# Local attention of a fused attention and feed-forward kernel, cut into blocks of 26 queries and 32 keys in place of 58 and 64

## The reference

```python
B, H, S, D = 4, 8, 576, 64; factor = 4
out_d = sm_attn(q_d, k_d, v_d)           # q, k, v averaged over groups of 4 rows: 144 positions
out_up = np.repeat(out_d, factor, axis=2)
mask = np.abs(pos[:, None] - pos[None, :]) < factor
scores = scale * np.matmul(q, k.transpose(0, 1, 3, 2))
scores = np.where(mask, scores, -1000000000.0)
attn = softmax(scores)                    # max taken off, exp, divided by the row's sum
out_local = np.matmul(attn, v)
return out_up + out_local
# then x (2304 tokens, 512 wide): h = x @ w_in (1024), h * softmax(h), layer norm * g_ln, @ w_out
# then h = x @ w_in2 (2048), h * cos(h), @ w_out2
```

## Time and profile before

| | us |
|---|---|
| median of three runs | 696.54 (693.97 to 698.17) |
| profiled execution, its own time | 697.5 |
| span of the profiled execution, first to last instruction | 695.7 |
| TensorE matmuls busy | 680.9 (98%) |
| VectorE, ScalarE, GpSimd busy | 440.8, 407.6, 233.3 |

### The profile page before, as it was taken

How to read it: one execution, slowest core, us unless ns; L and a number is a source line. 1 busy time by engine, 2 the same in 40 slices (tenths; PEclk the granted TensorE clock), 3 DMA queues, 4 the chain that set the end, 5 groups by cost and what they waited for, 6 DMA issues and landing times.

```text
span 695.7 us, 12769 instructions
## 1 busy us (share of the span) xinstructions
PE 680.9 (98%) x4783; PEld 601.3 (86%) x4783; DVE 440.8 (63%) x806; ACT 407.6 (59%) x849; POOL 233.3 (34%) x315
## 2 busy tenths in 40 slices
PE   7889999999999999999999999999999999999998
PEld 4567889889889999999898988888989898899986
DVE  7688964664662424266888888975555676655553
ACT  4558874664654665565666657564444676444444
POOL 6697864454542455411222255700000430000000
PEclk9999999999999999999999999999999999999999
DMA  8944222231300000537544343342222336322202
GB/s 286 319 139 148 77 82 70 79 107 41 100 1 1 1 1 1 181 137 257 202 168 158 124 171 147 120 183 106 106 107 106 114 125 244 137 109 106 106 1 90
DMA packets 18446, 82.77 MB, mean 119 GB/s; under 512 B 1873, under 2 KB 5969, under 8 KB 15057
## 3 DMA queue, kind: packets, MB, share of 16 engines
q1 hardware_dynamic: 18384, 81.96, 33.6%
HBM read 62.56 MB, written 19.40 MB: 118 GB/s over the span
## 4 chain that ended last, share of the span: by engine, by line
PE 91%; POOL 3%; DVE 2%; issue 2%; ACT 0%; POOLq 0%; ACTq 0%
PE ps L1586 28%; PE ps L1563 25%; PE ps L1419 15%; PE ps L1450 14%; PE ps L1434 2%; PE ps L1391 1%; PE ps L1329 1%; PE ps L1377 1%; PE ps L1366 1%; POOL vpairs L519 1%; DVE xT L1123 1%; POOL qgT L501 1%; DVE turn L1264 1%; PE ps L1322 1%; PE ps L1351 1%
## 5 line engine op out<-in xcount | busy, mean ns | idle before, releaser
L1563 PE MATMUL ps<-y_parts,w_parts 128*128 128x384 f32 x1008 | 203.2, 336 | 0.7 <-ACT part L942 0.7
L1563 PEld LDWEIGHTS ps<-y_parts,w_parts 128*128 128x128 f32 x1008 | 180.4, 188 | 15.8 <-ACT part L942 1.1
L1586 PE MATMUL ps<-wo,g_hi 128*128 128x512 f32 x576 | 179.2, 392 | 0.0
L1586 PEld LDWEIGHTS ps<-wo,g_hi 128*128 128x128 f32 x576 | 105.8, 188 | 11.8
L1586 PE MATMUL ps<-wo,g_lo 128*128 128x512 f32 x288 | 114.3, 397 | 0.0
L956 ACT ACTIVATE turn<-h,quarter 128x384 f32<-128x384 f32 x96 | 59.0, 615 | 79.6 <-DVE h L1256 79.3
L1450 PE MATMUL ps<-ln_hi,w_split 128*128 128x384 f32 x384 | 103.3, 339 | 0.0
L1270 DVE TENSOR_TENSOR turn<-h,turn 128x384 f32<-128x384 f32 x96 | 61.7, 643 | 43.9 <-ACT turn L962 43.9
L1256 DVE TENSOR_TENSOR h<-ps,part 128x384 f32<-128x384 f32 x72 | 40.1, 557 | 56.8 <-PE ps L1563 56.6
L1419 PE MATMUL ps<-w_split,x_hi 128*128 128x512 f32 x288 | 73.1, 396 | 0.1
L606 POOL TENSOR_TENSOR y_parts<-xT,y_parts 128x768 fp32r<-128x768 f32 x17 | 32.8, 1944 | 117.5 <-ACT y_parts L831 117.5
(11 more groups left out here) (110 smaller groups left out, 974.1 us busy)
## 6 DMA issues: line engine op xcount, KB each, us to landing
w_parts<-w_kept SPq DMA_DIRECT2D x16, 1792.0 KB, 7.4
w_kept<-w_parts SPq DMA_DIRECT2D x8, 1792.0 KB, 6.7
qk_in<-in_qk SPq DMA_DIRECT2D x16, 586.0 KB, 4.3
vblk<-in_v_blocks SPq DMA_DIRECT2D x16, 384.0 KB, 5.1
v<-in_v_rows SPq DMA_DIRECT2D x16, 288.0 KB
result<-o_sb SPq DMA_DIRECT2D x18, 256.0 KB, 3.7
xT<-in_w_in SPq DMA_DIRECT2D x8, 512.0 KB, 7.8
raw_wo<-in_w_out SPq DMA_DIRECT2D x8, 512.0 KB, 5.7
```

Of the source, the lines that this page charges most:

```text
L1563: last = nc.tensor.matmul(product_ps(s, k), w[:, m, a, c, :], y_parts[:, n, b, c, :], start=(not adds and c == 0 and m == 0 and n == 0), s ...
L1586: last = nc.tensor.matmul(o_ps(tile), g[n][:, t * P:(t + 1) * P], wo[:, p, w, f, :], start=(first and m == 0), stop=(done and m == 2))
```

## The change

Blocks shrink to 32 keys and 26 queries; there are 23. In `scores` block j now uses 32 columns of the array, 32(j mod 4), and the 64 rows of its head: eight tiles. In `results` a block's 32 keys stand in a quarter of the rows (r) and the head in half of the columns: again eight tiles. Result slots s = j // 4 go to banks s mod 4, four banks in place of two, at column 160 and up; slot 2 shares bank 2 with the coarse result and so comes last and waits for `gout_copied`. As a bank of the results is now also the bank of the coarse scores, `group_scores` waits for `out_added` too. The local probabilities are 2 x 6 x 32 = 384 wide (were 640) and take three transposes and one copy. Buffers, mask and input layout follow.

```diff
-KEYS = 64
+KEYS = 32
-SLOTS = NBLK // 2
+SLOTS = -(-NBLK // 4)
-PIECE = 2 * BLK
-LAST = S - 4 * PIECE
+PIECE = 4 * BLK
+LAST = S - (SLOTS - 1) * PIECE
+RESULTS = 160
 def t_order(i):
-    return (1, 3, 0, 2) if i > 1 else (0, 2, 1, 3)
+    return (1, 2, 0) if i > 1 else (0, 1, 2)
+        def result_ps(i, s, first, count):
+            at = RESULTS + s // 4 * PIECE + first
+            return ps[:, pair_banks(i) + s % 4, at:at + count]
 # scores
                 for j in range(NBLK):
-                    a, s = j % 2, j // 2
+                    a, s = j % 4, j // 4
 # group_scores
                 need(pe, gout_copied, was + 1)
+                need(pe, out_added, 3 * (was + 1))
 # transpose_probs, x == 0
-                    need(pe, prT_copied, 4 * (before_in_banks(i) + 1))
-                    for m in range(4):
+                    need(pe, out_added, 3 * (before_in_banks(i) + 1))
+                    for m in range(3):
 # results
-                for j in range(NBLK):
-                    a, s = j % 2, j // 2
+                for j in sorted(range(NBLK), key=lambda j: j // 4 == 2):
+                    a, s = j % 4, j // 4
                     count = min(BLK, S - j * BLK)
+                    if j == 8:
+                        pe.wait_ge(gout_copied, i + 1)
                     for h in range(2):
-                        m = 2 * h + s // 2 if s < SLOTS - 1 else 4 + h
-                        keys = slice(s % 2 * KEYS, (s % 2 + 1) * KEYS)
-                        at = s // 2 * PIECE + a * BLK
-                        last = nc.tensor.matmul(o_ps_pair(i, s % 2, at, count)[h * D:(h + 1) * D, :],
-                                                vblk[n][keys, h, a, s // 2, :],
-                                                prT[keys, m, a * KEYS:a * KEYS + count], start=True, stop=True)
+                        m, r = (h * SLOTS + s) // 4, (h * SLOTS + s) % 4
+                        keys = slice(r * KEYS, (r + 1) * KEYS)
+                        last = nc.tensor.matmul(result_ps(i, s, a * BLK, count)[h * D:(h + 1) * D, :],
+                                                vblk[n][keys, m, a, :], prT[keys, m, a * KEYS:a * KEYS + count],
+                                                start=True, stop=True)
 # add_scales: one operation over slots 0 to 3 (128 x 416), then slots 4 and 5 (104 and 56 columns)
 # start-up: the mask from two selects of 128 x 128 and four casts of 32 x 192 (were four selects and one cast)
```

More of the change, by code:

```diff
@@ L200, in two_scale_attention_moe @@
         v4 = [place(f"v4_{n}", [P, 4, FACTOR * D]) for n in range(2)]
-        vblk = [place(f"vblk{n}", [P, 2, 2, 3, D]) for n in range(2)]
+        vblk = [place(f"vblk{n}", [P, 3, 4, D]) for n in range(2)]
         vpairs = place("vpairs", [P, 4, 2 * D])
@@ L369, in two_scale_attention_moe @@
         o_stored = [sem(f"o_stored{n}") for n in range(6)]
-        lmax = slice(0, 10)
-        gneg, gsum, ginv = (slice(10 + 3 * n, 13 + 3 * n) for n in range(3))
+        lmax = slice(0, 2 * SLOTS)
+        gneg, gsum, ginv = (slice(2 * SLOTS + 3 * n, 2 * SLOTS + 3 * n + 3) for n in range(3))
         def pair_columns(pair, first, count):
@@ L609, in _ @@
             nc.gpsimd.memset(band[:], 0.0).then_inc(band_steps, 1)
[L610 to L618, removed]
+            for side, base in ((-1, 0), (1, 2 * PAD)):
+                pool.wait_ge(band_steps, 1 if side < 0 else 2)
+                nc.gpsimd.affine_select(out=band[:], in_=band[:], compare_op=ALU.is_ge, fill=MASKED, base=base,
+                                        pattern=[[-side, P]], channel_multiplier=side).then_inc(band_steps, 1)
             nc.gpsimd.memset(ident[:], 0.0).then_inc(ident_steps, 1)
@@ L711, in group_exp @@
                 act.wait_ge(gneg_ready, i + 1)
-                need(act, prT_ready, 4 * (i - 1))
+                need(act, prT_ready, 3 * (i - 1))
                 need(act, gsum_steps, 2 * (i - 1))
@@ L1117, in add_scales @@
                 dve.wait_ge(gout_copied, i + 1)
[L1118 to L1124, removed]
+                gn = PIECE // FACTOR
+                fine = ps[:, pair_banks(i):pair_banks(i) + 4, RESULTS:RESULTS + PIECE].rearrange("p s (g r) -> p s g r", r=FACTOR)
+                nc.vector.tensor_tensor(pair_columns(i, 0, 4 * PIECE).rearrange("p (s g r) -> p s g r", s=4, r=FACTOR), fine,
+                                        goT[:, 0:4 * gn].rearrange("p (s g) -> p s g", g=gn).unsqueeze(3).broadcast_to([P, 4, gn, FACTOR]),
+                                        ALU.add).then_inc(out_added, 1)
+                for s, count in ((4, PIECE), (5, LAST)):
+                    fine = result_ps(i, s, 0, count).rearrange("p (g r) -> p g r", r=FACTOR)
+                    coarse = goT[:, s * gn:s * gn + count // FACTOR]
+                    nc.vector.tensor_tensor(pair_columns(i, s * PIECE, count).rearrange("p (g r) -> p g r", r=FACTOR), fine,
+                                            coarse.unsqueeze(2).broadcast_to([P, count // FACTOR, FACTOR]),
                                             ALU.add).then_inc(out_added, 1)
[L1126 to L1129, removed]
             def split_in1(c):
@@ L1174, in _ @@
             nc.vector.tensor_copy(ident_bf[:], ident[:]).then_inc(ident_steps, 1)
-            dve.wait_ge(band_steps, 5)
-            nc.vector.tensor_copy(band_bf[:], band[:].unsqueeze(1).broadcast_to([P, SLOTS, KEYS])).then_inc(band_steps, 1)
-            dve.wait_ge(band_steps, 6)
+            dve.wait_ge(band_steps, 3)
+            for a in range(4):
+                rows = slice(a * KEYS, (a + 1) * KEYS)
+                nc.vector.tensor_copy(band_bf[rows], band[rows, rows].unsqueeze(1).broadcast_to([KEYS, SLOTS, KEYS])).then_inc(band_steps, 1)
+            dve.wait_ge(band_steps, 7)
             nc.vector.memset(band_bf[0:KEYS, 0, 0:PAD], MASKED).then_inc(band_steps, 1)
             past = S + PAD - (NBLK - 1) * BLK
-            nc.vector.memset(band_bf[KEYS:P, SLOTS - 1, past:KEYS], MASKED).then_inc(band_steps, 1)
+            a = (NBLK - 1) % 4
+            nc.vector.memset(band_bf[a * KEYS:(a + 1) * KEYS, SLOTS - 1, past:KEYS], MASKED).then_inc(band_steps, 1)
             sum_k(0)
@@ L1479, in _ @@
             transpose_probs(1, 1)
-            transpose_probs(1, 3)
+            transpose_probs(1, 2)
             keep_busy(2, 4)
@@ L1616, in laid_out @@
     padded[:, :, PAD:PAD + S, :] = v.reshape(PAIRS, 2, S, D)
-    blocks = np.zeros((PAIRS, 2, KEYS, 2, 2, 3, D), v.dtype)
+    blocks = np.zeros((PAIRS, 4, KEYS, 3, 4, D), v.dtype)
     for j in range(NBLK):
-        a, s = j % 2, j // 2
-        blocks[:, s % 2, :, :, a, s // 2, :] = padded[:, :, j * BLK:j * BLK + KEYS, :].transpose(0, 2, 1, 3)
+        for h in range(2):
+            place = h * SLOTS + j // 4
+            blocks[:, place % 4, :, place // 4, j % 4, :] = padded[:, h, j * BLK:j * BLK + KEYS, :]
     halves = w_in2.reshape(2, 2, P, 2, JOINS, P).transpose(4, 2, 0, 3, 1, 5)
```

77 lines of the change are left out of this document (32 added, 45 removed).

## The result

The changed kernel takes 724.34 us (median of 4 runs, 720.40 to 726.60) against 696.42 (693.97 to 698.17) beside it: 1.041 times as long, interval 1.038 to 1.044. The profiled execution took 726.6 us, its span 724.8, 29.1 more than before. Forecast were 706.5 and at most 717.5: the sign was right, the size was not.

A forecast was written before the change was run, and what follows sets the result against it. TensorE was taken to bound the kernel after the front, transfers before; results +9.0, wait +6.6, scores -3.3, transposes -2.6, transfers +0.3 gave 707.5 us, predicted as a median of 706.5; range 697.5 to 717.5, its own 703.5 to 710.

The forecast's parts named there:

- the sum: Whole kernel: results +9.0, wait +6.6, scores -3.3, transposes -2.6, transfers +0.3, together +10.0 us on the profiled 697.5.
- Front: Stretch up to the first `hidden`: larger transfers +0.3 us, mask start-up nothing; the forecast's terms there give +1.05 us.
- Queries and keys grow by 18 columns ... +0.3 us: Front transfers: 18 KB more a pair, 92 KB for five pairs at 245 to 382 GB/s, +0.3 us.
- Pairs 0 to 2 hide under transfers: Front: the longer results blocks of pairs 0 to 2 cost nothing, being covered by transfers.
- Scores: Local scores of pairs 5 to 15: smaller mask and shorter block, -0.30 us each, -3.3 us together.
- Eight tiles in turn, six matmuls or twelve passes each: ... 0.40 us: Local scores block: at 32 ns a pass it takes 0.40 us against 0.59.
- Rival 4: Results and scores: issue is the bound at 30 ns a matmul, scores +0.66 instead of -0.30 us; 717 us, chance 0.11.
- Results: Local results block: last start after 25 passes of 56 ns, 1.44 us, 0.75 more than before; +9.0 us together.
- The wait: Coarse scores now wait for VectorE's additions: 0.81 us in six iterations, 0.57 in three, +6.6 us together.
- Transposes: Local probabilities: three transposes fewer save 0.33 us a pair, counting for pairs 8 to 15, -2.6 us.
- The signs named beforehand: Profile rows: right if results about 1.6 us and scores about 0.6; wrong if results near 1.0 or 2.8, scores above 0.8.
- rivals 3 and 4: Third: no pass below 58 ns, scores save nothing, 709.8 us, chance 0.12; fourth: issue 30 ns a matmul, 717 us, 0.11.

The follow-up runs named there:

- a_quiet: Changed kernel with first-layer input weights and all loads behind them held until pair 1's results are done, output weights loaded later; 720.71 us (one run).
- a_rlw: Changed kernel with result matmuls in turn over six tiles, output weights loaded later and large filler matmuls in TensorE's idle time; 713.54 us, ratio 1.023.
- a_warm: Changed kernel with two large bf16 matmuls on zeros ahead of results of pairs 4 to 7 and coarse scores of pairs 5 to 8; 721.51 us.
- b_wait: Kernel before the change, with only the coarse scores' extra wait for the previous pair's additions (out_added) added; 703.38 us, ratio 1.010.
- a_robin: Changed kernel with its 46 result matmuls reordered so slots take turns and six tiles work at once; 717.59 us, ratio 1.030.
- a_w32: Changed kernel with 32 of 64 weight columns in the result matmuls (half the result rows omitted), plus eight zero matmuls at the start; 718.31 us (one run).

## Why the prediction was wrong

Of the 29.1 us, 9.9 were in the sum and 19.2 were not.

- **Front, the largest miss: +9.5 us against +1.05.** The step that failed is "Queries and keys grow by 18 columns ... +0.3 us" with "Pairs 0 to 2 hide under transfers". It counted the bytes of data and took more TensorE instructions as free under them. 1616 more records in pairs 0 to 15 are 13 more instruction packets, and in the front they share the full DMA engines that I had read in the earlier trace rows. Two stops, 7.0 us, are seen, and they are waits for such packets: stop and restart follow the count and the landing in each variant. That full DMA engines make the packets late is likely, not shown: a_quiet speaks for it, the first stop of a_rlw against it. The other 2.4 us are not separated. The front had 10.2 us more at 1.2 GHz than before; at the 0.35 us of a_warm's paragraph that would be 3.6 us, an estimate, so the clock can account for them. How long a stop lasts is partly luck: a_warm, without an edit in the front, had `hidden(0)` 2.1 us sooner than the kernel after, because its second stop lasted 2.1 us and not 4.45.
- **The clock, missing from the sum: about 4.8 us of the profiled execution.** The sum took all of t = 1 to 3 at full clock, because the kernel before had it. No rival had it either. The other terms, as measured, leave 4.5 us of the 9.3 to it, and a_warm at full clock was 4.8 us shorter. The size changes from one execution to the next: 1.2 us in a_quiet. Every run with the 46-matmul blocks has a mean clock of 0.990 or less, every run with the old blocks 0.995 or more, b_wait too, so it comes with the small matmuls and not with the wait alone. In a_robin, with the shorter block, t = 1 to 3 lost 5.4 us in place of 9.3, of which the block itself is 2.0. Which mix of small matmuls and idle time lowers the clock stays open.
- **Scores, mis-sized: -0.30 forecast, +0.07 measured, 11 pairs, 4 us.** The step is "Eight tiles in turn, six matmuls or twelve passes each: ... 0.40 us". The pass was right (32 ns), but eight tiles ask for a matmul every 8 ns and, behind the first 16, the issue gives one every 16.65. Rival 4 named this and I gave it 0.11. Its 30 ns were only an upper bound, as I wrote; from there I took the issue to cost nothing, where a value between nothing and 30 ns would have been the honest one, for the edit more than doubles the matmuls.
- **Results, right in kind, short in size: 1.652 us against 1.44, 11 pairs, 2.3 us.** The order of passes was as played through: slots start at 0, 267, 533, 800 and 1067 ns, and a_robin removed the queue. The load of 64 weight columns sets the pass (a_w32), as taken; but a pass is 58.4 ns and not 56, and each new pair of tiles adds about 33 ns; what makes these 33 ns is not shown.
- **The wait: right.** 0.86 us against 0.81 at a seam; 0.56 on average in t = 1 to 3 of b_wait against 0.57; nothing where `down` covers it. `gout_copied` showed no wait. In t = 0 the longer results hid behind VectorE as said (+0.49 against +0.51).
- **Transposes: right,** -0.33 us, read directly at t = 11, where only they and the results' +0.96 act.

The signs named beforehand said the same: the scores row of 0.99 us is above 0.8 (rivals 3 and 4), and the results row of 1.86 us lies above the 1.6 of the forecast.

For t = 4 to 11 the misses in size explain all: 8 x 0.21 for the results, 7 x 0.37 for the scores and 5 x 0.05 for the wait are 4.5 us, and measured minus forecast is 9.86 - 5.31 = 4.55.

## What to carry to other kernels

Small tiles of the array multiply instructions before they save time. Price each block three ways and take the largest: passes in a row in the busiest tile, by the weight columns that each loads; matmuls times the issue; and how the order spreads them over tiles. Then count the instructions as transfers that can come late wherever the DMA engines are busy, and look at what small matmuls do to the granted clock, in several executions and not in one.

## What the runs showed of the hardware that I had not expected

- A stop without any semaphore in the middle of a run of equal instructions was the instruction stream here. TensorE used a 16 KB packet for every 256 instructions or so, stopped for up to 5.1 us in a front with DMA shares of 0.9 to 1.1, and went on 1.3 to 1.6 us after the packet had landed.
- Float32 matmuls, two passes each, started every 16.65 ns when eight tiles took turns, the first 16 of a block within 163 ns. In t = 2, at the lowered clock, the same block took 0.95 us in place of 0.80.
- The granted clock differs between executions of the same instructions: t = 1 to 3 had 13.7 us at 1.2 GHz in the kernel after and 3.4 us in a_quiet, 9.3 and 5.7 us lost. One comparison of two executions can't tell an edit's effect on the clock from this.
